# A shared square for own and left-hand attention scores, and who empties the turned banks

## The chip, the cores and the metric

One core of one Trainium2 chip runs the whole program in one launch. The metric is device time in microseconds from start to end of an execution, lower is better. Its engines work through queues of their own, in order, and wait for one another on semaphores only: TensorE (PE), VectorE (DVE), ScalarE (ACT), GpSimd (POOL) and SyncE (SP), which here issues the loads.

## The reference

Attention with a window and sinks, then two gated or mixing layers. Cut to what the change touches:

```python
scores = scale * np.matmul(q, k.transpose(0, 1, 3, 2))     # B=2, H=8, S=768, D=64
is_sink = pos[None, :] < int(n_sink)                       # n_sink = 4
rel = pos[:, None] - pos[None, :]
keep = is_sink | ((rel >= 0) & (rel < int(window)))        # window = 128
scores = np.where(keep, scores, -1000000000.0)
a = np.exp(scores - np.max(scores, axis=-1, keepdims=True))
a = a / (np.sum(a, axis=-1, keepdims=True) + 1e-09)
x = np.matmul(a, v)
# then h = relu(x @ w_in), halves u and v, v normalised, w_spatial @ v + b, u * v, @ w_out
# then a token mixer (w_tok1, w_tok2) and a channel mixer (w_ch1, w_ch2), each added to its input
```

Everything is float32. Products that need its precision are done as three products of a rounded high half and a low half (hi x hi, hi x lo, lo x hi); scores take the query once, with its halves stacked over the partitions, against k_hi and k_lo.

## The kernel before

**Tiles and heads.** The queries are cut into 12 tiles of 128 rows, six for each of the two sequences, and a tile has 8 heads: 96 heads in all, numbered n = 8t + h. In the text i is t modulo 6, the place in the sequence. A query of a tile can see its own tile's keys up to itself, keys of the tile to the left that lie after its own place (window 128), and the sinks. So a head scores 288 columns: 128 own, 128 left-hand, and 32 between them that hold the sinks. At i = 0 it scores only its own 128. The keys lie in `k_hi` and `k_lo` as two squares around the sink columns; even tiles overwrite the first, odd tiles the second, so own and left-hand change places from tile to tile.

**One head, step by step.** All engines walk the same numbered steps n, each with its own list for a step.
- TensorE, `score(n)`: two products (high and low keys) into one of two score banks; it waits until the mask step of head n-2 is done.
- VectorE, `mask_scores(n)` (L780): one fused step adds the mask to the bank, writes `masked` and takes the row's least value, since scores are negated. The profile shows it as a custom operation and an accumulator read.
- ScalarE, `exps(n)` (L611): exp(-(masked) + least) into `probs`.
- TensorE, `turn_pair(m)` at step 2m+3: transposes the squares of heads 2m and 2m+1 against the identity into one of two banks (L989). Two squares a head, so four transposes; at i = 0 one a head, so two.
- `pair_out(m)` copies the bank into `p_t`: ScalarE for even m (L627), VectorE for odd m (L788), 512 columns.
- TensorE, `values(m)` at step 2m+5: each square of `p_t` times 66 columns of V of its tile (64, a one for the sum, a zero), L1023. One such product shows as two records in the trace.
- Sinks: every fourth step ScalarE gathers the sink columns of four heads into `p_cat` (L619), TensorE turns them (L997) straight after the pair of odd m, ScalarE copies them out (L635), and one product adds their values (L1031).
- VectorE, `x_out(g)`, at steps divisible by 4, straight after the mask step: sum, reciprocal and product (L795, L797, L801) give `x_nat`.
- TensorE, `turn_x(t)` at step 8t+13: transposes x (L1005). ScalarE and VectorE split it into `x_hi` and `x_lo` (L642, L807).

**The two turn banks.** Pairs, sinks and x take them in turn, in the order of `TURNS`; before it writes a bank TensorE waits (`wait_turn_bank`) until what was turned two places earlier is copied out. In step 8t+13 the order is pair (odd m), sinks, x: x waits for the copy of that pair.

**Preparation.** For a group of four heads, ScalarE rounds the queries (`q_high`, L586) at n % 4 == 1 and VectorE makes their low halves (`q_low`, L769) at n % 4 == 2. The keys' high halves come from GpSimd (L515; the first two from ScalarE), their low halves from GpSimd (L517), both in `k_prepare` at n % 4 == 0, for the next group.

**Filler.** Quarters of the first layer's products (`first_quarters`, L950 to L952) are put between the attention's products on TensorE by the table `WINDOWS`, in units of four quarters: one unit in tiles 2 and 3, two in tiles 4, 5, 7, 8, 10 and 11, three in 6 and 9. ScalarE empties them (`first_out`). VectorE takes the moments of v at steps with n % 8 in (3, 7) and normalises it there, GpSimd takes the root and splits it (L548, L550). The order inside a step is written out by hand; there is no planner.

**After the attention** the rest of the filler, the spatial product, the output product and the two mixers run, TensorE-bound and with their own lines; the change does not touch them.

## Time and profile before

| | us |
|---|---|
| median of 3 runs (lowest to highest) | 509.32 (509.27 to 510.44) |
| the profiled execution | 509.37 |
| its span | 507.5 |
| TensorE busy | 492.1 (97%) |
| VectorE busy | 211.1 (42%) |
| ScalarE busy | 163.5 (32%) |
| GpSimd busy | 171.0 (34%) |

The span runs from the first to the last instruction; the execution's time has 1.9 us around it. The trace names engines PE (matmul), PEld (its weight load), DVE, ACT, POOL, SP. The number behind L is the line of the kernel. The granted TensorE clock is 0.999 on average. The shares are means over very different parts: in the attention part VectorE and ScalarE are two to four times as busy as behind it.

In a row of the timeline a span is an instruction's duration from start to end. Instructions of one engine overlap: the next can start before the end of the one in front, so what an instruction takes of its queue is the distance to the next start, where nothing is waited for.

### The profile page before, as it was taken

Reading aid. Unit: us, or ns where it says so; the run is one execution under the profiler, and the core shown is the slowest. Engines: PE = TensorE matmul, PEld = TensorE weight load, DVE = VectorE, ACT = ScalarE, POOL = GpSimd, SP = SyncE. Lnnn points to the kernel's source line nnn. Section 1 sums busy time; section 2 is a strip of 40 time slices with the busy share of each in tenths; the row PEclk is TensorE's granted clock in tenths of the full one; section 3 lists DMA queues with packets and bytes.
Section 4 is the critical chain, followed back from the end, with each engine's and each line's share of the span. In section 5 each row is a group of like instructions: output and inputs, shape, how many; then the busy total and the mean of one; then the engine's idle time right before and its main releaser. Section 6 shows DMA issues by size and latency. Waiting matters only on the chain.

```text
span 507.5 us, 7154 instructions
## 1 busy us (share of the span) xinstructions
PE 492.1 (97%) x2664; PEld 436.1 (86%) x2664; DVE 211.1 (42%) x527; ACT 163.5 (32%) x343; POOL 171.0 (34%) x185
## 2 busy tenths in 40 slices
PE   3899999999999999999999999999999999999997
PEld 2788989999999899999888898888888888888885
DVE  5577777677676416754222232112131131211212
ACT  5577656565556242112342232010010010010010
POOL 3655653654451488701305057970000000000000
PEclk9999999999999999999999999999999999999999
DMA  7455322432311134300202013420020000100002
GB/s 238 150 166 170 112 77 86 137 118 91 106 43 33 61 96 134 89 0 1 77 1 65 19 45 102 136 72 0 1 83 1 0 1 0 70 14 0 1 0 83
DMA packets 19189, 34.03 MB, mean 67 GB/s; under 512 B 2256, under 2 KB 4560, under 8 KB 19152
## 3 DMA queue, kind: packets, MB, share of 16 engines
q1 hardware_dynamic: 19008, 33.55, 21.1%
q8 instruction: 22, 0.36, 0.3%
q14 instruction: 15, 0.12, 0.1%
q10 hardware_dynamic: 144, 0.00, 0.0%
HBM read 30.39 MB, written 3.15 MB: 66 GB/s over the span
## 4 chain that ended last, share of the span: by engine, by line
PE 89%; POOL 4%; DMA 2%; DVE 2%; issue 2%; ACT 1%; SPq 0%; ACTq 0%; POOLq 0%; DVEq 0%
PE bank L950 24%; PE bank L951 24%; PE bank L952 24%; PE bank L1023 6%; PE bank L989 3%; PE bank L965 2%; PE bank L966 2%; PE bank L1031 1%; PE bank L1182 1%; PE bank L1005 1%; POOL win_lo L539 1%; POOL k_lo L517 1%; DMA stage<-w_in 1%; DMA stage<-w_sp 1%; POOL wsp_lo L539 1%
## 5 line engine op out<-in xcount | busy, mean ns | idle before, releaser
L939 DVE SCALAR_TENSOR_TENSOR hch_lo<-bank,hch_hi 128x512 fp32r<-128x512 f32 x36 | 24.9, 692 | 153.8 <-ACT hch_hi L728 153.8
L728 ACT ACTIVATE hch_hi<-bank 128x512 fp32r<-128x512 f32 x36 | 21.5, 598 | 169.0 <-PE bank L952 169.0
L611 ACT ACTIVATE probs<-masked,small 128x288 f32<-128x288 f32 (+1 forms) x96 | 49.0, 512 | 49.5 <-DVE small L780 49.2
L780 DVE CUSTOM_DVE_ANT_0 masked<-bank,masks 128x288 f32<-128x288 f32 (+1 forms) x96 | 41.0, 428 | 38.9 <-PE bank L966 33.8
L952 PE MATMUL bank<-up_hi,wc_lo 128*128 128x512 f32 x144 | 56.0, 389 | 0.0
L951 PE MATMUL bank<-up_lo,wc_hi 128*128 128x512 f32 x144 | 56.0, 389 | 0.0
L950 PE MATMUL bank<-hch_hi,wc_hi 128*128 128x512 f32 x144 | 56.0, 389 | 0.0
L951 PE MATMUL bank<-hch_lo,wc_hi 128*128 128x512 f32 x144 | 56.0, 389 | 0.0
L950 PE MATMUL bank<-up_hi,wc_hi 128*128 128x512 f32 x144 | 56.0, 389 | 0.0
L952 PE MATMUL bank<-hch_hi,wc_lo 128*128 128x512 f32 x144 | 56.0, 389 | 0.0
L1023 PE MATMUL bank<-v_sl,p_t 128*128 128x66 f32 x352 | 46.8, 276 | 0.0
L1023 PEld LDWEIGHTS bank<-v_sl,p_t 128*128 128x128 f32 x352 | 45.8, 199 | 0.4
L965 PE MATMUL bank<-k_hi,q_st 128*128 128x288 f32 (+1 forms) x96 | 35.4, 371 | 10.1 <-DVE q_st L769 8.0
L517 POOL TENSOR_TENSOR k_lo<-k_raw,k_hi 128x512 fp32r<-128x512 f32 x24 | 34.0, 1415 | 5.8 <-ACT k_hi L579 4.0
L950 PE MATMUL bank<-wsp_hi,vn_hi 128*128 128x384 f32 x96 | 32.1, 335 | 0.9 <-POOL vn_lo L550 0.9
L951 PE MATMUL bank<-wsp_lo,vn_hi 128*128 128x384 f32 x96 | 32.1, 334 | 0.0
L952 PE MATMUL bank<-wsp_hi,vn_lo 128*128 128x384 f32 x96 | 32.1, 334 | 0.0
L952 PEld LDWEIGHTS bank<-up_hi,wc_lo 128*128 128x128 f32 x144 | 27.0, 188 | 5.7
L952 PEld LDWEIGHTS bank<-hch_hi,wc_lo 128*128 128x128 f32 x144 | 27.0, 188 | 5.7
L950 PEld LDWEIGHTS bank<-hch_hi,wc_hi 128*128 128x128 f32 x144 | 27.1, 188 | 5.6
L951 PEld LDWEIGHTS bank<-up_lo,wc_hi 128*128 128x128 f32 x144 | 27.0, 188 | 5.6
L951 PEld LDWEIGHTS bank<-hch_lo,wc_hi 128*128 128x128 f32 x144 | 27.0, 188 | 5.6
(121 smaller groups left out, 1022.7 us busy)
## 6 DMA issues: line engine op xcount, KB each, us to landing
k_raw<-kT SPq DMA_DIRECT2D x24, 256.0 KB, 3.1
q_raw<-qT SPq DMA_DIRECT2D x24, 256.0 KB, 2.9
stage<-w_c SPq DMA_DIRECT2D x24, 256.0 KB, 2.7
v_sl<-vL SPq DMA_DIRECT2D x12, 264.0 KB, 2.9
outT<-out_sb SPq DMA_DIRECT2D x12, 256.0 KB, 2.1
stage<-w_sp SPq DMA_DIRECT2D x12, 192.0 KB, 2.5
stage<-w_in SPq DMA_DIRECT2D x8, 256.0 KB, 3.6
stage<-w_out SPq DMA_DIRECT2D x4, 256.0 KB, 3.2
```

Of the source, the lines that this page charges most:

```text
L517: pool.tensor_tensor(k_lo[:, hs, c0:c0 + P], raw, k_hi[:, hs, c0:c0 + P], ALU.subtract).then_inc(k_ready, 1)
L539: pool.tensor_tensor(lo, staged(n), hi, ALU.subtract).then_inc(w_lo_ready, 1)
L611: act.activation(probs[:, n % N_PROB, 0:w], masked[:, n % N_MASKED, 0:w], ACT.Exp, bias=least[:, n % 8:n % 8 + 1], scale=-1.0).then_inc(ex ...
L728: act.activation(hch_hi[:, u[2] % N_HCH, :], bank[:, :], ACT.Relu).then_inc(hi_ready, 1)
L780: dve.tensor_tensor_reduce(masked[:, n % N_MASKED, 0:w], score_bank[n % 2][:, 0:w], masks[:, m:m + w], 1.0, 3e38, ALU.add, ALU.min, least[ ...
L939: dve.scalar_tensor_tensor(out=hch_lo[:, f % N_HCH, :], in0=bank[:, :], scalar=0.0, in1=hch_hi[:, f % N_HCH, :], op0=ALU.max, op1=ALU.subt ...
L950: pe.matmul(out, a_hi, b_hi, start=first, stop=False, skip_group_check=skip)
L951: pe.matmul(out, a_hi, b_lo, start=False, stop=False, skip_group_check=skip)
L952: return pe.matmul(out, a_lo, b_hi, start=False, stop=last, skip_group_check=skip)
L965: pe.matmul(score_bank[n % 2][:, 0:w], q, k_hi[:, h, 0:w], start=True, stop=False)
L989: ins = pe.transpose(tr_bank[n % 2][:, at_:at_ + P], probs[:, head % N_PROB, c:c + P], ident[:, :])
L1023: ins = pe.matmul(bank[:, DV * place:DV * place + DV], p_t[:, m % N_PT, at_:at_ + P], v_sl[:, slot, DV * h:DV * h + DV], start=m % 2 == 0 ...
```

## The change

For the tiles with i of 2 and more, `merged(t)`, an entry of the square is own where the key lies at or below the query's place, and left-hand above: the two triangles fill one square exactly. The kernel after makes use of that.
- VectorE copies the own triangle over the left-hand square in the score bank (`copy_predicated`), waits for that on `own_placed`, and runs the fused mask step over the square and the sinks, 160 columns. ScalarE's exp has the same 160 columns.
- `turn_pair` turns one square per head. `pair_out(m)` is on ScalarE for every m and copies 256 columns. A step later VectorE writes, beside it in `p_t`, the square times a triangle of ones (`own_triangles`, SBUF to SBUF).
- `values(m)` multiplies the whole square by V of the left-hand tile and the own triangle by `v_diff`, own V minus left-hand V, which GpSimd makes (`value_difference`, twice a tile).
- At i = 1 the scores skip the sink columns: 256 in place of 288. There the turned bank holds four squares as before; VectorE copies the second head's (`second_head`), and ScalarE, after it, the first head's. At i = 0 ScalarE copies the 256 columns of every pair.
- The keys' high halves move from GpSimd to ScalarE, at n % 4 == 0, behind the other work of that step.
- Two triangles and a square mask are made at the start, and one mask fewer is written by ScalarE. Buffers are laid out anew.

```diff
@@ mask and slot geometry
+def merged(t):
+    return t % NT >= 2
+def in_bank(t):
+    i = t % NT
+    return slice(0, P) if i == 0 else slice(0, SLOT) if i == 1 else slice(0, P + SINKS) if i % 2 else slice(P, BAND)
+def squares(t):
+    i = t % NT
+    return [0] if i == 0 else [0, P] if i == 1 else [0] if i % 2 else [P]
+HALVED = [m for m in range(N_PAIR) if m // 4 % NT]
...
@@ gpsimd
-                if g >= 2:
-                    pool.wait_ge(s_k[g % 2], 16 * (g // 2 + 1))
-                    if g >= 4:
-                        pool.wait_ge(scored, 4 * (g - 1))
-                    pool.tensor_scalar(k_hi[:, hs, c0:c0 + P], raw, 1.0, 1.0, ALU.mult, ALU.mult).then_inc(k_high_done, 1)
...
+            def value_difference(t, half):
+                cols = slice(GV * half, GV * half + GV)
+                pool.wait_ge(s_v[t % 3], 16 * (t // 3 + 1))
+                pool.wait_ge(s_v[(t - 1) % 3], 16 * ((t - 1) // 3 + 1))
+                pool.wait_ge(valued, 4 * (t - 1) + 2 * half + 2)
+                pool.tensor_tensor(v_diff[:, cols], v_sl[:, t % 3, cols], v_sl[:, (t - 1) % 3, cols], ALU.subtract)\
+                    .then_inc(diff_ready, 1)
...
+                if n % 4 == 1 and (n // 8, n % 8 // 4) in diff_n:
+                    value_difference(n // 8, n % 8 // 4)
@@ scalar
             def pair_out(m):
-                cols = 2 * P * len(blocks(m // 4))
                 act.wait_ge(turned, turn_index[("pair", m)] + 1)
+                if m in halved_n and not merged(m // 4):
+                    act.wait_ge(pt_own, halved_n[m])
...
-                act.activation(p_t[:, m % N_PT, 0:cols], tr_bank[turn_index[("pair", m)] % 2][:, 0:cols], ACT.Copy)\
+                act.activation(p_t[:, m % N_PT, 0:2 * P], tr_bank[turn_index[("pair", m)] % 2][:, 0:2 * P], ACT.Copy)\
                    .then_inc(pt_act, 1)
...
-                for m in range(0, N_PAIR, 2):
+                for m in range(N_PAIR):
...
+                if n % 4 == 0 and 2 <= n // 4 + 1 < N_GROUP:
+                    k_high(n // 4 + 1)
@@ vector
+                if merged(t):
+                    own, previous = (odd, even) if t % 2 else (even, odd)
+                    dve.copy_predicated(previous, tri_own.bitcast(U32), own).then_inc(own_placed, 1)
                 if n >= N_MASKED:
                     dve.wait_ge(exped, n - N_MASKED + 1)
-                dve.tensor_tensor_reduce(masked[:, n % N_MASKED, 0:w], score_bank[n % 2][:, 0:w], masks[:, m:m + w],
+                if merged(t):
+                    dve.wait_ge(own_placed, placed_n[n])
+                dve.tensor_tensor_reduce(masked[:, n % N_MASKED, cols], bank[:, at_], masks[:, m:m + at_.stop - at_.start],
                                          1.0, 3e38, ALU.add, ALU.min, least[:, n % 8:n % 8 + 1]).then_inc(masked_ready, 1)
...
+            def second_head(m):
+                dve.wait_ge(turned, turn_index[("pair", m)] + 1)
...
+                dve.tensor_copy(p_t[:, m % N_PT, 2 * P:4 * P], tr_bank[turn_index[("pair", m)] % 2][:, 2 * P:4 * P])\
+                   .then_inc(pt_own, 1)
+            def own_triangles(m):
+                whole, own = p_t[:, m % N_PT, 0:2 * P], p_t[:, m % N_PT, 2 * P:4 * P]
+                dve.wait_ge(pt_act, m + 1)
+                dve.tensor_tensor(own.rearrange("p (h c) -> p h c", c=P), whole.rearrange("p (h c) -> p h c", c=P),
+                                  tri_turned.unsqueeze(1).to_broadcast([P, 2, P]), ALU.mult).then_inc(pt_own, 1)
...
-                for m in range(1, N_PAIR, 2):
-                    if turn_step(m) == n:
-                        pair_out(m)
+                for m in HALVED:
+                    if turn_step(m) == n and not merged(m // 4):
+                        second_head(m)
+                    if turn_step(m) == n - 1 and merged(m // 4):
+                        own_triangles(m)
@@ tensor
-                if kind == "pair" and m % 2 == 0:
-                    pe.wait_ge(pt_act, m // 2 + 1)
-                if kind == "pair" and m % 2 == 1:
-                    pe.wait_ge(pt_dve, m // 2 + 1)
+                if kind == "pair":
+                    pe.wait_ge(pt_act, m + 1)
...
+                pe.wait_ge(pt_act, m + 1)
+                if m in halved_n:
+                    pe.wait_ge(pt_own, halved_n[m])
+                if (t, g % 2) in diff_n and m % 2 == 0:
+                    pe.wait_ge(diff_ready, diff_n[t, g % 2])
...
+                    if t % NT == 0:
+                        parts = [(P * n, v_sl[:, t % 3, :])]
+                    elif t % NT == 1:
+                        parts = [(2 * P * n, v_sl[:, (t - 1) % 3, :]), (2 * P * n + P, v_sl[:, t % 3, :])]
+                    else:
+                        parts = [(P * n, v_sl[:, (t - 1) % 3, :]), (2 * P + P * n, v_diff)]
```

## Rows read from the trace of the kernel before

**Rows 1.** The page, chain of waits, shares of the span by engine.
```profile
PE 89%; POOL 4%; DMA 2%; DVE 2%; issue 2%; ACT 1%; SPq 0%; ACTq 0%; POOLq 0%; DVEq 0%
```

**Rows 2.** Busy time in one stretch: bounds, length, each engine's us (x instructions), clock, DMA.
```profile
50.60:64.10 13.50, 13.50 (x98) 12.56 (x97) 10.51 (x31) 9.00 (x20) 7.83 (x8) 1.00 0.36 117
```

**Rows 3.** Timeline, tile 10: start us, us, engine, line, operation, out<-in, shape, count.
```profile
141.00 0.30 PE L965 MATMUL bank<-k_hi,q_st 128*128 128x288 f32 x1
...
141.13 0.29 PE L966 MATMUL bank<-k_lo,q_st 128*128 128x288 f32 x1
...
141.96 0.60 PE L989 MATMUL bank<-ident,probs 128*128 128x128 f32 x4
...
142.39 1.00 PE L1023 MATMUL bank<-v_sl,p_t 128*128 128x66 f32 x8
```

**Rows 4.** Groups by form: xcount | busy us, mean ns | idle before, releaser.
```profile
L780 DVE CUSTOM_DVE_ANT_0 masked<-bank,masks 128x288 f32<-128x288 f32 x80 | 36.4, 455 | 32.2 <-PE bank L966 27.3 <-issue 4.3
...
L780 DVE CUSTOM_DVE_ANT_0 masked<-bank,masks 128x128 f32<-128x128 f32 x16 | 4.6, 290 | 6.7 <-PE bank L966 6.4
...
L611 ACT ACTIVATE probs<-masked,small 128x288 f32<-128x288 f32 x80 | 42.7, 534 | 41.9 <-DVE small L780 41.7
...
L611 ACT ACTIVATE probs<-masked,small 128x128 f32<-128x128 f32 x16 | 6.3, 398 | 7.5 <-DVE small L780 7.5
...
L627 ACT ACTIVATE p_t<-bank 128x256 f32<-128x256 f32 x4 | 1.5, 369 | 0.0
...
L515 POOL TENSOR_SCALAR k_hi<-k_raw 128x512 fp32r<-128x512 f32 x22 | 14.1, 639 | 36.1 <-PE bank L966 36.1
```

**Rows 5.** Timeline, tile 10, from scores of head 84 to the x transposes.
```profile
143.54 0.49 PE L965 MATMUL bank<-k_hi,q_st 128*128 128x288 f32 x1
...
144.20 0.46 DVE L780 CUSTOM_DVE_ANT_0 masked<-bank,masks 128x288 f32<-128x288 f32 x1 [1.56 <-PE bank L966]
...
144.58 0.16 DVE L795 TENSOR_SCALAR small<-bank 128x4 f32<-128x4 f32 x1
...
144.77 0.18 DVE L797 RECIPROCAL small<-small 128x4 f32<-128x4 f32 x1
...
144.98 0.42 DVE L801 TENSOR_TENSOR x_nat<-bank,small 128x256 f32<-128x256 f32 x1
...
145.33 0.45 DVE L780 CUSTOM_DVE_ANT_0 masked<-bank,masks 128x288 f32<-128x288 f32 x1
...
145.82 0.54 ACT L611 ACTIVATE probs<-masked,small 128x288 f32<-128x288 f32 x1 [0.38 <-DVE small L780]
...
145.94 0.69 DVE L788 COPY p_t<-bank 128x512 f32<-128x512 f32 x1 [0.16 <-PE bank L989]
...
146.26 0.26 ACT L635 ACTIVATE p_ts<-bank 128x128 f32<-128x128 f32 x1
...
146.69 0.65 PE L1005 MATMUL bank<-ident,x_nat 128*128 128x128 f32 x4
```

**Rows 6.** Timeline, tile 9, the same two instructions of TensorE.
```profile
128.66 0.49 PE L965 MATMUL bank<-k_hi,q_st 128*128 128x288 f32 x1
...
132.34 0.60 PE L1005 MATMUL bank<-ident,x_nat 128*128 128x128 f32 x4
```

**Rows 7.** Timeline, end of tile 8 and start of tile 9.
```profile
117.30 0.38 PE L965 MATMUL bank<-k_hi,q_st 128*128 128x288 f32 x1
...
121.39 0.46 DVE L780 CUSTOM_DVE_ANT_0 masked<-bank,masks 128x288 f32<-128x288 f32 x1
...
122.34 0.29 ACT L619 ACTIVATE p_cat<-probs 128x128 f32<-128x128 f32 x1
...
123.10 0.27 PE L997 MATMUL bank<-ident,p_cat 128*128 128x128 f32 x1
```

**Rows 8.** Timeline, start of tile 5, TensorE.
```profile
70.73 0.30 PE L997 MATMUL bank<-ident,p_cat 128*128 128x128 f32 x1 [0.42 <-ACT p_cat L619]
```

**Rows 9.** VectorE's low halves of the queries, min/median/max ns.
```profile
L769 DVE SCALAR_TENSOR_TENSOR q_st<-q_raw,q_st x24: 689/690/1079, 6.3 to 154.9; 64x512 fp32r<-64x512 f32 x24
```

More of the change, by code:

```diff
@@ L175 @@
 COLS = E_ID + P
-assert all(at % P == 0 for at in (A_V, A_PROBS, A_PT, A_PTS, A_CAT, A_X, B_X, X_SLOT, B_WIN, C_VN, D_U, E_V, E_STAGE, E_ID))
+assert H * DV <= 5 * P
+assert all(at % P == 0 for at in (A_V, A_DIFF, A_PROBS, A_PT, A_PTS, A_CAT, A_X, B_X, X_SLOT, B_WIN, C_VN, D_U, E_V, E_STAGE, E_ID))
 A_WSP = 0
@@ L210, in build @@
         banks = [ctx.enter_context(nc.psum_tensor(f"bank{i}", [P, 512], F32)) for i in range(8)]
-        k_hi = at("k_hi", A_K_HI, [H, BAND], F32R)
-        k_lo = at("k_lo", A_K_LO, [H, BAND], F32R)
+        k_hi_flat = at("k_hi", A_K_HI, [H * BAND + SINKS], F32R)
+        k_lo_flat = at("k_lo", A_K_LO, [H * BAND + SINKS], F32R)
+        k_hi, k_lo = (flat[:, 0:H * BAND].rearrange("p (h c) -> p h c", h=H) for flat in (k_hi_flat, k_lo_flat))
         q_st = at("q_st", A_Q, [2, 512], F32R)
@@ L219, in build @@
         vs_sl = at("vs_sl", A_VS, [2 * GV])
[L220 to L221 removed]
+        v_diff = at("v_diff", A_DIFF, [H * DV])
+        masked = at("masked", A_MASKED, [N_MASKED, SLOT])
+        probs = at("probs", A_PROBS, [N_PROB, SLOT])
         p_t = at("p_t", A_PT, [N_PT, 512])
@@ L227, in build @@
         scratch = at("mask_scratch", B_X + X_SLOT, [8, P])
-        rel_sb, key_sb, diag_keep, prev_keep, sink_keep, first_keep, second_keep = (scratch[:, i, :] for i in range(7))
+        rel_sb, key_sb, diag_keep, prev_keep, sink_keep, first_keep, second_keep, square_keep = (scratch[:, i, :] for i in range(8))
+        tri_own, tri_turned = masks[:, TRI_OWN:TRI_OWN + P], masks[:, TRI_TURNED:TRI_TURNED + P]
         x_hi = [at(f"x_hi{i}", B_X + X_SLOT * i, [KT, HALF], F32R) for i in range(2)]
@@ L959, in score @@
                     pe.wait_ge(k_ready, g + 1)
-                if h == 0 and t % NT == 1:
+                if h == 0 and t % NT == 2:
                     pe.wait_ge(ks_ready, t // NT + 1)
@@ L964, in score @@
                 q = q_st[:, g % 2, P * (n % 4):P * (n % 4) + P]
-                pe.matmul(score_bank[n % 2][:, 0:w], q, k_hi[:, h, 0:w], start=True, stop=False)
-                pe.matmul(score_bank[n % 2][:, 0:w], q, k_lo[:, h, 0:w], start=False, stop=True).then_inc(scored, 1)
+                high, low, out = k_hi[:, h, :], k_lo[:, h, :], score_bank[n % 2][:, 0:BAND]
+                if t % NT == 0:
+                    high, low, out = k_hi[:, h, 0:P], k_lo[:, h, 0:P], score_bank[n % 2][:, 0:P]
+                if t % NT == 1:
+                    high, low = beside_sinks(k_hi_flat, h), beside_sinks(k_lo_flat, h)
+                    out = score_bank[n % 2][:, 0:2 * P].rearrange("p (b c) -> p b c", b=2)
+                pe.matmul(out, q, high, start=True, stop=False)
+                pe.matmul(out, q, low, start=False, stop=True).then_inc(scored, 1)
             def wait_turn_bank(n):
@@ L987, in turn_pair @@
                     pe.wait_ge(exped, head + 1)
-                    for c, _ in blocks(m // 4):
+                    for c in squares(m // 4):
                         ins = pe.transpose(tr_bank[n % 2][:, at_:at_ + P], probs[:, head % N_PROB, c:c + P], ident[:, :])
@@ L1014, in values @@
                     pe.wait_ge(x_nat_ready, g - 1)
-                if m % 2 == 0:
-                    pe.wait_ge(pt_act, m // 2 + 1)
-                else:
-                    pe.wait_ge(pt_dve, m // 2 + 1)
-                at_ = 0
-                for head in (2 * m, 2 * m + 1):
-                    h, place = head % H, head % 4
-                    for _, slot in blocks(t):
+                pe.wait_ge(pt_act, m + 1)
[3 more added lines that the diff above has]
+                    pe.wait_ge(diff_ready, diff_n[t, g % 2])
+                first = m % 2 == 0
+                for n in range(2):
+                    h, place = (2 * m + n) % H, (2 * m + n) % 4
+                    if t % NT == 0:
+                        parts = [(P * n, v_sl[:, t % 3, :])]
[3 more added lines that the diff above has]
+                        parts = [(P * n, v_sl[:, (t - 1) % 3, :]), (2 * P + P * n, v_diff)]
+                    for at_, v in parts:
                         ins = pe.matmul(bank[:, DV * place:DV * place + DV], p_t[:, m % N_PT, at_:at_ + P],
-                                        v_sl[:, slot, DV * h:DV * h + DV], start=m % 2 == 0 and at_ == 0, stop=False,
-                                        skip_group_check=True)
-                        at_ += P
+                                        v[:, DV * h:DV * h + DV], start=first, stop=False, skip_group_check=True)
+                        first = False
                 if ("sink", g) in turn_index and m % 2:
```

78 lines of the change are left out of this document (43 added, 35 removed).

## Prediction

> **What bounds the kernel now.** I read the chain of waits first: TensorE holds 89% of it, VectorE 2% and ScalarE 1% [rows 1]. Whatever shortens TensorE's queue can therefore shorten the whole, as long as no other queue comes to release it. Next the table by stretches [rows 2]: the change touches the attention part alone, and there TensorE has no idle time (13.50 of 13.50 us around tile 4), while VectorE is busy for 10.51 and ScalarE for 9.00 us. So TensorE bounds, but VectorE's queue is full to 78%, and it works in a fixed order: it has little room to be late. The granted clock is 1.00 there, so I price nothing for the clock. The form table [rows 4] gives the durations, and three stretches of the timeline [rows 5 to 7] tell how close VectorE and ScalarE come to releasing TensorE. They are the part of the profile that decides here.
>
> **The change part by part.**
>
> *Transposes.* In the eight tiles with i from 2 to 5 (tiles 2 to 5 and 8 to 11) each head turns one square in place of two: 64 transposes go. Four of them take from 141.96 to 142.39 us on TensorE, 0.43 us, or 0.1075 each [rows 3]: 64 x 0.1075 = 6.9 us off. The value products stay at two a head, since the second now multiplies the own triangle by V_own minus V_prev. The tiles with i = 1 score 256 columns in place of 288, 32 products shorter by 32 columns each. A product of 288 columns releases the queue after some 0.13 us (141.00 to 141.13 us [rows 3]), so 32 columns are about 0.014 us and all 32 products 0.4 us. Half of them lie in the start phase, where TensorE waits anyway. I take 0.2. Together 7.1 us off, so 502.3 us is the floor if nothing new is waited for.
>
> *VectorE's mask step.* Before, one fused add and minimum over 288 columns, 0.455 us, after which the next instruction starts 0.38 us behind its start (144.20 to 144.58) [rows 4, 5]. Now a predicated copy of 128 columns within the score bank, a wait for it on the engine's own semaphore, then the fused step over 160 columns. The slope of the fused step is (455 - 290)/160 = 1.03 ns a column [rows 4], so 128 columns fewer take 0.13 us off: 0.38 becomes 0.25. No row shows a predicated copy, nor VectorE writing a bank. Bounds: 0.16 us, the time of an operation on four columns out of a bank, and 0.42, one of 256 columns out of a bank [rows 5]. The nearest row is the 128-column form of the fused step, also out of a bank, 0.29 [rows 4]. I take that, and 0.03 for the wait on itself (the gap in 144.58 + 0.16 to 144.77, where the next instruction waits in the same way). A mask step is then 0.32 + 0.25 = 0.57 in place of 0.38: 0.19 longer, 64 times.
>
> *Own triangles.* 32 products over 256 columns in SBUF take the place of 20 bank copies of 0.69 (two each in these eight tiles, 16 of the 20). The 256-column product at 144.98 takes 0.42 and lets the next start after 0.35 [rows 5]. VectorE as a whole: 8 x 0.19 + 4 x 0.35 - 2 x 0.60 = 1.7 us more a tile, 10.51 to 12.2 us against a tile of 13.50 - 0.86 = 12.6 for TensorE. It still fits in sum; what is lost is lost where the order makes TensorE wait.
>
> *ScalarE.* It gets 22 high halves of keys (from GpSimd, 0.64 each there [rows 4]), one more bank copy per four heads at 0.37 for 256 columns, and shorter exponentials (136 ns over 160 columns, so 0.11 less each [rows 4]). The key half is issued after exp(n) and the gather of a step n divisible by 4, 0.6 us before exp(n+1), which waits longer than that for VectorE's mask, so it is hidden. If VectorE were early it would cost up to 0.6 at each group. GpSimd gives up 14 us and gets 16 value differences; TensorE reads them a good four steps after they can start, so they are free.
>
> *The wait that I expect to bind: the x transposes.* In step 8t+13 TensorE turns pair, sinks and then x in alternate banks, so x waits until the pair's bank is emptied. Before, VectorE did that straight behind mask(n). Now ScalarE does it behind exp(n), which waits for mask(n). Walk through tile 10, n-1 = 84, n = 85 [rows 5]: mask(84) starts at 144.20 and takes 0.57, the own triangles 0.35, the three operations of x_out 0.75 as before (144.58 to 145.33), so mask(85) starts at 145.87 and not 145.33. Its fused step starts 0.32 later, at 146.19; exp(85) started 0.49 behind a fused step of 288 columns (145.33 to 145.82), so 0.36 behind this one: 146.55. ScalarE's next instruction came 0.44 behind exp (145.82 to 146.26), now 0.33: 146.88. + 0.37 bank copy = 147.25, + 0.06 (146.63 to 146.69) = 147.31. TensorE would otherwise be there at 146.69 - 0.22 = 146.47. Loss 0.84 us. All eight x turns of merged tiles have this order. Tile 9 has one more unit of filler: its x turn comes 132.34 - 128.66 = 3.68 us behind the start of the pair's scores, that of tile 10 after 146.69 - 143.54 = 3.15, so it loses 0.84 - 0.53 = 0.3 [rows 5, 6]. Sum 7 x 0.84 + 0.3 = 6.2 us.
>
> *Ends of tiles.* In the last two steps of a tile VectorE does two masks, x_lo, q_low and the moments. In tile 8 they keep it until mask(72) can start at 121.39 [rows 7]. It grows by 2 x 0.19 + 0.35 = 0.73, so mask(72) starts 121.39 - 117.30 + 0.73 = 4.82 us behind the scores of step 70. Gather ended 1.24 behind mask(72)'s start, now 0.19 - 0.11 more, 1.32: 6.14. TensorE wants the gathered columns 123.10 - 117.30 = 5.80 behind those scores, less 0.44 for four transposes: 5.36. Loss 0.8. Tile 10 has the same row pattern, 0.8. At the end of tile 4 it already waits 0.42 for the gather [rows 8]: there the delay of 0.81 is paid in full and the 0.44 aren't won, 1.25. Three ends with more cover (3, 5, 9) I put at 0.3 each. Sum 3.8 us.
>
> *Start.* Three of the key halves that leave GpSimd come before the filler starts, where GpSimd's low halves of weights set the pace; ScalarE gets the same work between its exponentials. Bounds -1.9 (three halves of 0.64 off GpSimd [rows 4]) and +1.9 (the same three on ScalarE); I take +0.3, since ScalarE's queue feeds the next scores.
>
> **Sum.** - 7.1 + 6.2 + 3.8 + 0.3 = + 3.2 us. The profiled execution took 509.37 us with a span of 507.5, and the median of the runs is 509.32, so one number serves both: 509.4 + 3.2 = **512.6 us**, slower by 0.6%.
>
> *A rule against the change.* Own triangles read two operands in SBUF. VectorE's q_low does that already: mostly 0.69 us, at worst 1.08 [rows 9]. The Trainium skill ("SBUF — State Buffer", section "SBUF: two separate sides") says that such an operation and a GpSimd one that reads SBUF take a shared port pair in turn, and that the loser blocks for the whole instruction; what it gives is a rival, below.
>
> **Rivals.**
>
> A, no change (508.8 to 510.4). Only the x turns cost, the tile ends have cover that I don't see in [rows 7]: 509.4 - 7.1 + 6.2 + 0.3 = 508.8, with one end paid 509.6. For it: VectorE has time left over in sum. Against: [rows 7, 8] show it late at the ends already.
>
> B, faster, about 506.7. The predicated copy is at its lower bound of 0.16: 0.13 less per mask, 2 x 8 masks before x turns and 3 x 6 at tile ends, 34 x 0.13 = 4.4, which gives 508.2, and the start wins 1.2 net of the key halves. It decides from a copy under some 0.2 us. For it: GpSimd is relieved where the start needs it. Against: the 128-column row at 0.29 [rows 4].
>
> C, slower by more, 516 to 517. The own triangles lose their slot to GpSimd or the copy takes 0.42: 34 x 0.13 = 4.4 gives 517.0. If GpSimd holds it back as it does q_low, a product of own triangles waits up to 0.39 (1.08 - 0.69 [rows 9]) in the 14 places where it is on the path; with GpSimd at work in two thirds of them 9 x 0.39 = 3.5, 516.1. For it: the long rows of q_low. Against: at the x turn GpSimd now waits for ScalarE's key half, so it is mostly idle there. The port rule of that page is this case, at the price that the rows allow.
>
> D, the transposes go but the order never binds (x finds its bank free): 502.3 to 504. It would need mask(85) to end 0.84 us sooner than the walk, which no row supports.
>
> **How the numbers follow.** Forecast 0.42, A 0.19, B 0.15, C 0.18, D 0.06. The range from 505.0 to 517.5 leaves out D and the far side of C, and takes both ends of the unknown copy; the forecast's own is 511 to 514.5. A measurement of this kernel tells 0.3%, 1.5 us, from no change: faster (under 507.8) 0.22, same 0.20, slower (over 510.9) 0.58.
>
> **What would show it.** In the profile after: 112 transposes of probs and not 176, at 0.11 us each; a predicated copy near 0.29, 64 times; TensorE waiting for ScalarE's copy of p_t ahead of the x transposes, some 0.8 us, seven or eight times; waits for p_cat at starts of tiles 5, 9 and 11; key halves on ScalarE beside no wait of TensorE for k_lo. I am wrong if x transposes follow the value products without a gap, if the copy is far from 0.3, or if the stretch before 29 us moves by over 1.2 us.

## The result, and the profile after

| | before | after |
|---|---|---|
| median (lowest to highest), us | 509.88 (509.27 to 510.88) | 524.15 (523.89 to 524.64) |
| span of the profiled execution | 507.5 | 522.3 |
| TensorE busy | 492.1 | 496.0 (95%) |
| VectorE busy | 211.1 | 221.6 (42%) |
| mean granted clock | 0.999 | 0.993 |

The ratio is 1.028 [1.026, 1.030]: slower by 14.3 us, or 14.8 by span, where 3.2 were forecast. The sign held; the size did not, and the time lies outside the range.

The chain of waits after, shares by engine; VectorE had 2% in [rows 1].

```profile
PE 80%; DVE 11%; issue 4%; ACT 2%; DMA 2%; POOL 0%; DVEq 0%; SPq 0%; ACTq 0%
```

So VectorE's queue now holds some 57 us of that chain (11% of 522) in place of 10. The stretches of the profile after say where TensorE lost time: bounds, length, busy us of PE, PEld, DVE, ACT and POOL, granted clock, DMA share, GB/s. In [rows 2] PE was never idle at clock 1.00.

```profile
43.00:56.00 13.00, 10.86 (x64) 8.86 (x63) 8.07 (x34) 7.62 (x21) 6.83 (x7) 0.95 0.30 93
56.00:70.00 14.00, 12.85 (x79) 11.22 (x77) 11.68 (x40) 8.19 (x21) 6.57 (x6) 0.92 0.29 87
70.00:84.00 14.00, 13.57 (x82) 12.46 (x82) 10.40 (x34) 6.89 (x19) 7.26 (x8) 0.88 0.18 60
```

TensorE is idle for 2.1 of 13 us around tile 3. The clock figures are means of two levels: in the trace it goes to the lower one, 1.2 GHz, twice, for 3.4 us each, at 54.7 and at 71.8 us. The length of each tile, from the start of its first scores to the next tile's (the last: to head 95), read off the two timelines:

| tile | 0 | 1 | 2 | 3 | 4 | 5 | 6 | 7 | 8 | 9 | 10 | 11 |
|---|---|---|---|---|---|---|---|---|---|---|---|---|
| before | 9.7 | 12.1 | 12.2 | 12.5 | 13.9 | 14.6 | 13.6 | 11.6 | 13.2 | 15.9 | 13.9 | 11.5 |
| after | 9.4 | 13.4 | 13.1 | 16.3 | 16.8 | 15.0 | 14.1 | 11.4 | 14.7 | 16.5 | 15.1 | 13.1 |

The eight merged tiles carry 12.9 us of the 14.1, tiles 3 and 4 alone 6.6. From head 95 to the first spatial product it is 0.7 us more (25.1 before, 25.8 after), and from that product on nothing changed (320.5 and 320.6). What TensorE waits for in the attention (engine, line, releaser; us in all, times, longest). The PEld rows are the weight load's side of the same waits, so they don't add to the PE rows; "issue" means that the profile shows no releaser:

```profile
PEld bank L1074 <- issue: 9.0, 13, 1.4
PE bank L1074 <- ACT p_cat L667: 5.9, 9, 1.1
PEld bank L1082 <- ACT p_t L677: 4.5, 8, 0.9
PE bank L1082 <- ACT p_t L677: 3.4, 7, 0.8
```

L1074 is the transpose of the gathered sinks, L1082 that of x. The x transposes wait seven times, as forecast, six times for 0.40 to 0.48 us and once for 0.78; the gather costs more than they do, where before its waits made 0.7 us in two places, one of them in [rows 8]. The added work by form:

```profile
L834 DVE COPY_PREDICATED bank<-masks,bank 128x128 f32<-128x128 uint32 x64 | 18.6, 291 | 21.7 <-PE bank L1045 21.1
L839 DVE CUSTOM_DVE_ANT_0 masked<-bank,masks 128x160 f32<-128x160 f32 x64 | 20.8, 325 | 10.0 <-DVE bank L834 1.1
L854 DVE TENSOR_TENSOR p_t<-p_t,masks 128x256 f32<-128x256 f32 x32 | 15.4, 480 | 0.5 <-ACT p_t L677 0.4
L821 DVE SCALAR_TENSOR_TENSOR q_st<-q_raw,q_st 64x512 fp32r<-64x512 f32 x24 | 20.5, 855 | 3.1 <-ACT q_st L635 2.4
L628 ACT ACTIVATE k_hi<-k_raw 128x512 fp32r<-128x512 f32 x24 | 14.8, 616 | 1.9 <-DMA k_raw<-kT 1.9
```

The copy takes 0.29 us as priced. But VectorE stands idle for 10.0 us ahead of the 64 fused steps. The timeline of tile 10's step with the x transpose, after, against [rows 5]:

```profile
155.28 0.49 PE L1044 MATMUL bank<-k_hi,q_st 128*128 128x288 f32 x1
...
155.93 0.29 DVE L834 COPY_PREDICATED bank<-masks,bank 128x128 f32<-128x128 uint32 x1
...
156.37 0.33 DVE L839 CUSTOM_DVE_ANT_0 masked<-bank,masks 128x160 f32<-128x160 f32 x1
...
157.70 0.29 DVE L834 COPY_PREDICATED bank<-masks,bank 128x128 f32<-128x128 uint32 x1
...
158.13 0.32 DVE L839 CUSTOM_DVE_ANT_0 masked<-bank,masks 128x160 f32<-128x160 f32 x1
...
158.50 0.43 ACT L659 ACTIVATE probs<-masked,small 128x160 f32<-128x160 f32 x1 [0.61 <-DVE small L839]
...
158.83 0.36 ACT L677 ACTIVATE p_t<-bank 128x256 f32<-128x256 f32 x1
...
159.25 0.66 PE L1082 MATMUL bank<-ident,x_nat 128*128 128x128 f32 x4 [0.43 <-ACT p_t L677]
```

Every link of the walk is there, in order. The x transpose starts 3.97 us behind the scores, where 3.77 were walked. The difference is in the step from copy to fused step: 0.44 and not 0.32, twice. In 62 of the 64 heads it is 0.42 to 0.44; the other two, 0.78 and 0.86, stay unexplained. The next runs are about that, and about what the rest costs.

### The profile page after: what moved, and what is told of

It is laid out like the page before. It is cut to its first block, busy times and chain, and to the rows that moved or that the text cites. A ratio compares the mean times of both kernels' runs of the same rounds, so it can differ in the third digit from the quotient of the medians.

```text
span 522.3 us, 7207 instructions
## 1 busy us (share of the span) xinstructions
PE 496.0 (95%) x2600; PEld 433.2 (83%) x2600; DVE 221.6 (42%) x608; ACT 169.5 (32%) x386; POOL 168.8 (32%) x179
## 4 chain that ended last, share of the span: by engine, by line
PE 80%; DVE 11%; issue 4%; ACT 2%; DMA 2%; POOL 0%; DVEq 0%; SPq 0%; ACTq 0%
PE bank L1019 22%; PE bank L1021 22%; PE bank L1020 22%; PE bank L1107 5%; DVE masked L839 2%; DVE q_st L821 2%; DVE bank L834 2%; PE bank L1044 2%; PE bank L1082 1%; PE bank L1045 1%; PE bank L1066 1%; PE bank L1265 1%; DVE p_t L854 1%; DMA stage<-w_sp 1%; DVE small L881 1%
## 5 line engine op out<-in xcount | busy, mean ns | idle before, releaser
L659 ACT ACTIVATE probs<-masked,small 128x160 f32<-128x160 f32 (+2 forms) x96 | 41.9, 436 | 61.0 <-DVE small L839 59.6
L553 POOL TENSOR_TENSOR k_lo<-k_raw,k_hi 128x512 fp32r<-128x512 f32 x24 | 30.6, 1274 | 73.5 <-ACT k_hi L628 69.4
L1044 PE MATMUL bank<-k_hi,q_st 128*128 128x288 f32 (+2 forms) x96 | 35.9, 375 | 10.7 <-DVE q_st L821 8.7
L839 DVE CUSTOM_DVE_ANT_0 masked<-bank,masks 128x160 f32<-128x160 f32 (+2 forms) x96 | 32.0, 335 | 24.6 <-PE bank L1045 11.6
L1107 PE MATMUL bank<-v_sl,p_t 128*128 128x66 f32 x224 | 39.7, 286 | 0.5 <-DVE p_t L854 0.3
L1107 PEld LDWEIGHTS bank<-v_sl,p_t 128*128 128x128 f32 x224 | 34.9, 208 | 3.1 <-issue 1.1
L1044 PEld LDWEIGHTS bank<-k_hi,q_st 128*128 128x128 f32 x96 | 20.1, 209 | 14.9 <-issue 7.1
```

The costliest lines, as they stand in the source:

```text
L553: pool.tensor_tensor(k_lo[:, hs, c0:c0 + P], raw, k_hi[:, hs, c0:c0 + P], ALU.subtract).then_inc(k_ready, 1)
L659: act.activation(probs[:, n % N_PROB, cols], masked[:, n % N_MASKED, cols], ACT.Exp, bias=least[:, n % 8:n % 8 + 1], scale=-1.0).then_inc( ...
L839: dve.tensor_tensor_reduce(masked[:, n % N_MASKED, cols], bank[:, at_], masks[:, m:m + at_.stop - at_.start], 1.0, 3e38, ALU.add, ALU.min, ...
L1044: pe.matmul(out, q, high, start=True, stop=False)
L1107: ins = pe.matmul(bank[:, DV * place:DV * place + DV], p_t[:, m % N_PT, at_:at_ + P], v[:, DV * h:DV * h + DV], start=first, stop=False, s ...
```

## The experiments

All ratios are against the kernel before, run on the same chip. A gain or loss in us is the difference of two medians. The kernel before itself had medians from 509.29 to 510.37 on these chips, so a difference between runs of different chips can be off by some 0.5 to 1 us. Against the kernel before on its own chip, the change lost 14.3 us, run 3 10.0, run 4 5.6, run 8 7.1 and run 11 6.2.

**1. The saving alone** (before, merged tiles turn one square a head).

```diff
-                    for c, _ in blocks(m // 4):
+                    for c, _ in blocks(m // 4)[0:1 if m // 4 % NT >= 2 else 2]:
```

> The kernel before, with one change: in the tiles with i of 2 and more each head turns one square instead of two (64 transposes fewer). The banks are still copied in their full 512 columns and all four value products are made, so the second square's product works on old data: that part of the computation is left out. Theory (TensorE bounds, and what it saves comes back): 64 x 0.1075 = 6.9 us off, 509.9 to 503.0 us. Rival (the transposes were hidden behind the other engines anyway): 508 us or more. If VectorE and ScalarE hold TensorE at some places even so, it lies between, near 505.

506.49 us, ratio 0.994 [0.993, 0.996]: 3.2 us, under half of 6.9, and between the expectation's two theories. TensorE, done sooner, now waits for the gather four times, 2.0 us, where it was 0.7 in two:

```profile
PE bank L997 <- ACT p_cat L619: 2.0, 4, 0.9
```

The old kernel was bound by TensorE, but its feeders were hardly earlier.

**2. Without the copy and its wait** (the left-hand scores stay in place of the own).

```diff
-                    dve.copy_predicated(previous, tri_own.bitcast(U32), own).then_inc(own_placed, 1)
...
-                if merged(t):
-                    dve.wait_ge(own_placed, placed_n[n])
```

> The kernel after without the predicated copy and the wait for it: the mask step is the fused operation over 160 columns alone, the own scores are left out of the square. The trace of after shows 0.44 us from the start of that copy to the start of the fused step (0.32 predicted), 64 times. Theory (the lengthened mask step is what makes VectorE late, and TensorE waits for what follows it): most of the 14 us go, 524.2 to 508 or less (505 if TensorE is back to back again). Rival (the key halves and bank copies on ScalarE hold it): at most 4 us off, 520 or more. Rival (the own triangles' products and GpSimd's port): 515 to 518.

509.75, ratio 1.000 [0.999, 1.001]: 14.4 us better than the change, which is the whole loss. But the copy isn't the only cost: against run 1, which also turns fewer squares, 3.3 us remain. GpSimd is in part of them: TensorE waits for the own triangles four times, 1.3 us in all. One of them:

```profile
147.93 1.29 POOL L594 TENSOR_TENSOR vn_lo<-v_sb,vn_hi 128x512 fp32r<-128x512 f32 x1
148.03 0.08 DVE L836 DVE_READ_ACCUMULATOR2_ANT small<- 128x1 f32 x1
148.03 1.47 DVE L851 TENSOR_TENSOR p_t<-p_t,masks 128x256 f32<-128x256 f32 x1
...
149.65 0.41 PE L1104 MATMUL bank<-v_sl,p_t 128*128 128x66 f32 x2 [0.36 <-DVE p_t L851]
```

The own triangles take 1.47 us in place of 0.42: they start behind GpSimd's product of two SBUF operands and end 0.28 us after it (149.22), and TensorE waits for them. The Trainium skill ("SBUF — State Buffer", section "SBUF: two separate sides") describes this lock, taken for a whole instruction; the row agrees.

**3. ScalarE's bank copy ahead of its exponential** in merged tiles.

```diff
+                for m in range(N_PAIR):
+                    if turn_step(m) == n and merged(m // 4):
+                        pair_out(m)
...
-                    if turn_step(m) == n:
+                    if turn_step(m) == n and not merged(m // 4):
```

> The kernel after, with ScalarE's copy of the turned bank ahead of exp(n) in the step, not behind it, in the tiles with i of 2 and more. Theory (x transposes wait for the copy, which waits for exp and so for the mask): the 7.9 us of waits at the x transposes nearly go, since the copy can be done 0.7 us earlier; 524.2 to 518 or so, if the exponentials, 0.37 us later where ScalarE is behind, do not make the gather later. Rival (VectorE's queue decides wherever one looks, the x wait only takes over from the next wait): 523 to 525.

519.72, ratio 1.020 [1.018, 1.021]: 4.4 us back. The waits of the x transposes for `p_t` are gone and the clock is 1.000; the gather's are 6.7 us, where the change had 5.9, and the value products now wait for ScalarE's copy three times, 1.6 us. So the x term was real, at about 4.4 where 6.2 were forecast.

**4. The copy beside the scores, without a wait** (its result isn't used).

```diff
-                    dve.copy_predicated(previous, tri_own.bitcast(U32), own).then_inc(own_placed, 1)
+                    dve.copy_predicated(bank[:, BAND:BAND + P], tri_own.bitcast(U32), own).then_inc(own_placed, 1)
...
-                if merged(t):
-                    dve.wait_ge(own_placed, placed_n[n])
```

> The kernel after, with the predicated copy written to unused columns of the same bank, and the fused step not waiting for it: the copy's own time stays, the engine's wait for its result goes (the own scores are left out of the square). After shows 0.44 us from start to start, 0.29 of it the copy. Theory (the wait is 0.12 us longer than I priced and on the path in over 30 places): 524.2 to 517 to 519; the copy then takes 0.2 or so of the queue. Rival (the copy's own time is the whole price): 522 or more, and with the 509.8 of the run without a copy that splits the 14 us between copy and wait.

514.93, ratio 1.012 [1.010, 1.013]. Of the 14.4 us of run 2 the wait is 9.2 and the copy 5.2; with the kernel before of each chip taken off they are 8.6 and 5.6. The fused step now starts 0.20 us behind the copy's start in 49 heads, and 0.33 in the 15 whose copy follows the low halves of the queries directly.

**5. The copy into SBUF, wait kept.** The destination is `u_sb[:, 1, 3, S - P:S]`.

> The kernel after with the predicated copy written to unused columns of SBUF and not into the bank, the wait for it kept (the own scores are left out of the square). The wait cost 0.15 us behind the end of the copy and not the 0.03 I priced; the 0.03 came from writes to SBUF. Theory (it is writing the bank that makes the wait long): start to start falls from 0.44 to 0.32, and the time by 64 x 0.12 = 7.7 us of queue at 0.6, to 519 or 520. Rival (a wait for a 128-column copy costs that much wherever it writes): 0.44 and 524.

524.37, ratio 1.029 [1.027, 1.030]; still 0.44 from start to start. That it writes a score bank is not the cause.

**6. A plain copy, wait kept.**

```diff
-                    dve.copy_predicated(previous, tri_own.bitcast(U32), own).then_inc(own_placed, 1)
+                    dve.tensor_copy(previous, own).then_inc(own_placed, 1)
```

> The changed kernel with a plain copy in place of the predicated one (all 128 columns of every row are placed, so the scores are not the reference's); the wait for it stays. Theory 1, the late release belongs to the predicated copy (its wait lasts some 0.15 us behind the copy's end, where waits behind other instructions of this queue lasted 0.03): the fused step then starts 0.32 us behind the copy's start and not 0.44, 64 x 0.12 = 7.7 us of VectorE's queue, of which 0.6 counted in the run without the wait: -4.6 us, about 519.5. Theory 2, any operation that writes the score bank or is as short as this one releases its own engine as late: still 0.44, and 523.5 to 524.5.

525.82, ratio 1.030 [1.027, 1.033], 0.44 again. Nor is it the predicated form.

**7. A one-column copy takes the wait.**

```diff
                     dve.wait_ge(own_placed, placed_n[n])
+                    dve.tensor_copy(u_sb[:, 1, 3, S - 1:S], bank[:, 0:1])
```

> The changed kernel with a copy of one column (out of the score bank into SBUF) between the wait and the fused step, which so has a plain instruction ahead of it and no wait of its own for the copy. Theory 1, the fused step as the waiter is what pays (a wait ahead of it lasts 0.15 us behind the releasing instruction's end, and 0.03 ahead of ordinary ones): the small copy starts 0.32 us behind the predicated copy's start, the fused step some 0.06 to 0.1 behind that, 0.38 to 0.42 in all, and the time is 522 to 524. Theory 2, any instruction that waits for a 128-column operation on the bank starts as late: the small copy starts at 0.44, the fused step at 0.50 to 0.54, 64 x 0.08 x 0.6 = 3 us slower, about 527.

523.27, ratio 1.027 [1.024, 1.029]. The small copy starts 0.38 to 0.40 behind the predicated one in all 64, nearer to 0.44 than to 0.32, and the fused step 0.08 later. The waiting instruction isn't it either, or only by some 0.05.

**8. The wait for exp ahead of the copy**, so that one wait is left between the two.

```diff
                 if merged(t):
+                    if n >= N_MASKED:
+                        dve.wait_ge(exped, n - N_MASKED + 1)
...
-                if n >= N_MASKED:
+                if n >= N_MASKED and not merged(t):
```

> The changed kernel with the wait for the exponential (which frees the slot of masked) moved ahead of the predicated copy in merged tiles, so that one wait is left between copy and fused step. Theory 1, the second wait at this place is what takes the 0.12 us: 0.32 start to start, and about 519.5. Theory 2, it has long been served and costs nothing: still 0.44, and 523.5 to 524.5.

517.47, ratio 1.014 [1.012, 1.017]: 6.7 us back by moving a wait that had always been served. The timeline of this run:

```profile
147.67 0.30 DVE L836 COPY_PREDICATED bank<-masks,bank 128x128 f32<-128x128 uint32 x1 [0.82 <-PE bank L1047]
148.00 0.32 DVE L841 CUSTOM_DVE_ANT_0 masked<-bank,masks 128x160 f32<-128x160 f32 x1
```

0.33, and 0.31 to 0.34 in all 64: the 0.32 of the prediction. The profile after shows what was different (a line of the kernel, DVEq for VectorE's sequencer; count; min/median/max ns):

```profile
L838 DVEq EVENT_SEMAPHORE  x64: 21/21/21, 30.9 to 177.6; - x64
```

L838 is the wait for the copy. It became an instruction of its own, 64 times, while the wait for exp, written ahead of it, stands alone 28 times, all outside the merged tiles. The Trainium skill ("Perfetto Trace Analysis", section "Identifying Dependency Chains") says that an instruction that waits on multiple engines may get such instructions in front; the trace agrees with its 64, where one of the two engines is the instruction's own. In run 8 the exp wait has them and the wait for the copy none:

```profile
L834 DVEq EVENT_SEMAPHORE  x64: 21/21/1215, 28.9 to 170.8; - x64
```

The starts of these rows show where the 0.12 lies. In the kernel after, the separate wait starts 0.32 to 0.34 us behind the copy's start in all 64 heads, where in run 8 the fused step itself starts, and the fused step follows it 0.11 later (in 62 of them). Runs 5, 6 and 7 left this separate wait where it was (64 in each), so none of them could show this; in run 7 it stands ahead of the small copy, which starts 0.06 behind it.

Two waits as such are not dear: `x_nat` has two from tile 2 on, and starts 0.03 behind the reciprocal's end in all 24 instances, before and after. There it is the other, served wait that stands alone, and it starts 0.01 behind the reciprocal's start, so it is over before the reciprocal is:

```profile
L867 DVEq EVENT_SEMAPHORE  x20: 21/21/21, 45.0 to 185.1; - x20
```

So the 0.12 goes with a separate wait for the engine's own last result. That writing the two waits in the other order would do the same as run 8 follows from this, but wasn't tried.

**9. Copy and wait on the kernel before**, all else kept; the same without the wait.

```diff
+                if t % NT >= 2:
+                    dve.copy_predicated(score_bank[n % 2][:, BAND:BAND + P], ident[:, :].bitcast(U32),
+                                        score_bank[n % 2][:, 0:P]).then_inc(own_placed, 1)
...
+                if t % NT >= 2:
+                    dve.wait_ge(own_placed, sum(e // H % NT >= 2 for e in range(n + 1)))
```

> The kernel before, all its transposes and bank copies kept, with the predicated copy of 128 columns (into unused columns of the score bank, so the result is the reference's) and the wait for it ahead of the fused step in the 64 heads of merged tiles. Each mask step gets 0.44 us longer (0.29 copy + 0.15 wait). Theory 1, VectorE's queue sets the steps wherever an x transpose or a tile's end needs it (the 34 places of the prediction): 34 x 0.44 = 15 us, 524 to 526, the same as the whole change, although no transpose went. Theory 2, the kernel before has cover in each tile (VectorE 10.5 of 13.5 us), and 8 x 0.44 = 3.5 us a tile just eats it: under 517.

> The same without the wait: each mask step gets 0.20 us longer. Theory 1: 34 x 0.20 = 6.8 us, 516 to 517. Theory 2, cover: 510 to 512. Against the run with the wait it also gives the price of the wait at the old kernel's place: 0.24 x 64 = 15.4 us of queue, of which the changed kernel paid 9.2.

518.92, ratio 1.018 [1.016, 1.021], and 512.43, 1.004 [1.003, 1.006], against 510.16: 8.8 and 2.3 us. Both lie nearer to theory 2, cover, but above its figures: of the 28 us put into VectorE's queue 31% comes out at the end, of 12.8 a fifth. The first 0.2 us of a mask step nearly fit into the old kernel's cover, the next 0.24 cost 6.5. So the price of one more microsecond in that queue is not one factor: it rises as the cover is used up.

**10. Runs 3 and 4 together.**

> The changed kernel with two edits that were run alone before: ScalarE's bank copies ahead of its exponential (-4.4 us), and the predicated copy put beside the scores without the wait (-9.2 us; the copy's result is not used, so the scores of the later square are left out). Theory 1, the two lateness terms are paid in different places (x transposes here, tile ends there): they add, 524.15 - 13.6 = 510.5. Theory 2, both shorten one chain (mask, exponential, copy or gather, transpose), and what one has removed the other can't remove again: 512.5 to 514.5. Theory 3, the gaps of TensorE go, and with them its half-speed stretches and restarts: under 509.5.

515.51, ratio 1.011 [1.009, 1.013], run 4 within its uncertainty. They don't add: what run 3 won was lateness that the mask step had caused. That is theory 2, though its 512.5 to 514.5 was still too low.

**11. No product for the own triangles** (the second product takes the whole square).

> The kernel after without the own triangles' product: the second value product takes the whole square as well, so that part of the computation is left out. Theory: 32 x 0.35 us of VectorE's queue and all waits for the port in it go, so 516 to 518. If only the port waits mattered (2 us of the 15.4 us busy), 522.

515.53, ratio 1.013 [1.010, 1.015]: 8.6 us, about as much as the wait (run 4, on the same chip, has 514.93).

**12. The triangles elsewhere.** Between copy and fused step, on GpSimd, or (with run 3) a step later:

> The kernel after, with VectorE's own triangles issued between the predicated copy and the fused step of the mask, where the engine otherwise waits 0.15 us for its own copy; before they came behind the fused step. Theory (VectorE's queue is what is too long): 32 x 0.15 us less in the queue, of which what lies on the path comes back: 520 to 522. Rival (the mask of an even step itself is what is late, its result now comes 0.25 us later): 525 or more.

> The kernel after, with the own triangles' products made by GpSimd, ahead of its other work of a step. VectorE's queue loses 32 x 0.35 us and its exposure to GpSimd's port in that product. Theory (VectorE's queue decides): 0.35 us off at each of the 8 x turns and each of the tile ends, 524.2 to 518 or less, if GpSimd (24 us more for it) is in time. Rival (the shared port: one more GpSimd operation in each pair of steps blocks VectorE's q_low): 522 to 528, with long q_low rows.

> The kernel after with two reorderings: ScalarE's bank copy ahead of exp(n), as in the second experiment on order, which gave 519.7; and VectorE's own triangles behind the mask of the odd step, one step later, so that they no longer stand between mask(n) of an even step and mask(n+1). Theory (what counts is how late mask(n+1) of the first pair of a group is): 0.35 us off at x turns and gathers, some 16 places, 519.7 to 514 to 516, if TensorE's value products do not wait for the triangles in their place. Rival (VectorE's total is what counts): 519 to 520.

524.02 (ratio 1.030 [1.028, 1.031]), 532.35 (1.044 [1.040, 1.048]) and 569.51 (1.119 [1.117, 1.121]). The first fills the wait in some 25 heads (the next instruction starts 0.19 to 0.23 behind the copy) but wins nothing: the triangles take 585 ns on average there (480 in the change), VectorE waits 1.7 us for ScalarE's copies, which was 0.4, and TensorE waits for the gather 14 times, 9.3 us, in place of 9 times and 5.9. The fused step comes later in those heads, as the rival said. On GpSimd the triangles come too late for TensorE, and they hold VectorE's q_low up (mean 1008 ns, 855 in the change):

```profile
PE bank L1108 <- POOL p_t L559: 12.6, 10, 2.8
...
142.44 0.74 POOL L559 TENSOR_TENSOR p_t<-p_t,masks 128x256 f32<-128x256 f32 x1
...
142.66 1.06 DVE L831 SCALAR_TENSOR_TENSOR q_st<-q_raw,q_st 64x512 fp32r<-64x512 f32 x1
```

The 12.6 us of direct waits are the larger part; the expectation had made them a condition ("if GpSimd is in time") and priced only q_low. A step later on VectorE, the value products wait for them, far longer than I had expected:

```profile
PE bank L1110 <- DVE p_t L857: 30.6, 20, 2.4
```

**13. Key halves and value difference.** The high halves back on GpSimd (from the kernel after), or on ScalarE in the kernel before; and no `v_diff` (own V used).

> The kernel after, with the keys' high halves back on GpSimd as before (22 instructions of 0.64 us there, 0.62 on ScalarE). Theory (VectorE's mask step decides): within 1.5 us of 524.2, perhaps a gain of 1 at the start. Rival (ScalarE's longer queue is the cause): 515 to 519.

> The kernel before with one part of the change alone: the keys' high halves on ScalarE. Putting them back on GpSimd in the kernel after cost 7.3 us, and its trace has longer q_low rows on VectorE (0.96 us mean against 0.86). Theory (each GpSimd operation that reads SBUF lengthens VectorE's two-operand ones): q_low falls from 0.79 to 0.70 to 0.75 us mean, and the kernel wins 0.5 to 1.5 us. Rival (the seven microseconds came from the start or from GpSimd's lateness in the longer kernel): no change, or slower by the 0.6 us that ScalarE then takes in each group.

> The kernel after without GpSimd's value differences (16 operations, 13.6 us there); the second product takes the own values instead, so that part of the computation is left out. Theory of the shared port: VectorE's q_low and triangle rows get shorter (0.86 and 0.48 us mean now, 0.69 and 0.42 without GpSimd), 2 to 3 us of VectorE's queue, of which 0.5 to 0.6 per us lie on the path: 522.5 to 523. Rival (GpSimd's work moves no one): 524.

531.5 (1.042 [1.041, 1.044]), 509.34 (0.999 [0.999, 1.000]) and 523.73 (1.027 [1.025, 1.030]). Moving the key halves is worth 7.3 us in the new kernel and nothing in the old one; in the new one both the theory (within 1.5 us) and the rival (faster) missed. With them on GpSimd VectorE's products of two SBUF operands take longer (q_low mean 962 ns against 855, triangles 573 against 480) and TensorE's waits for them and for ScalarE's copies grow (10.3 against 8.7 us, 5.4 against 3.4). That the shared port alone does this is argued from these rows, not separated from GpSimd's later work. My expectation that q_low would get faster in the old kernel missed: mean 830 ns, 787 before. The value differences are free within the uncertainty, as priced, though the triangles get shorter without them (462 ns).

## Why the prediction missed

**The step that failed** is in *VectorE's mask step*: "and 0.03 for the wait on itself", from the gap behind an ordinary self-wait. The copy (0.29) and the fused step (0.25) were right. The wait lasts 0.12 longer, since the fused step had a wait already and the new one became an instruction of its own, which starts when the copy's result is there and puts the fused step 0.11 behind itself. The mask step is 0.69, not 0.57: 0.31 over before and not 0.19. Run 8 takes only that away and wins 6.7 us. The profile of before could have warned: there the wait for exp already stands as such an instruction 92 times, and I read no sequencer rows:

```profile
L779 DVEq EVENT_SEMAPHORE  x92: 21/21/1928, 11.0 to 161.9; - x92
```

**The transposes** are gone as forecast (112 at 0.11), but run 1 shows that they bring 3.2 us and not 6.9. An engine that finishes sooner meets its feeders sooner: the eight merged tiles got shorter by 0.2 to 0.8 us each, where 0.86 was due, and 0.7 of the 4.4 us won by head 95 were lost again before the first spatial product. I had counted that at the x turns and the ends alone.

The two can't be added up to the 11.6 us by which the span missed. Part of the 3.7 us stood in the sum under other names: 0.22 at each of eight x turns and 0.44 at three tile ends for TensorE's earlier arrival, 3.1 us. And they were measured in different kernels, where, as run 10 shows, such terms need not add. What is shown is that the mask step's longer wait is worth 6.7 us, over half of the miss.

**The x transposes** were late in the way that was walked, seven times, but their waits are 3.4 us in all, some 0.43 each where 0.84 was priced. Run 3 puts the term at 4.4 in place of 6.2.

**The ends of tiles.** Of the gather's nine waits, 5.9 us, five lie at ends of tiles and make 2.7 us, where 3.8 was forecast. The two that were walked came out: 0.76 and 0.78 for 0.8. The end of tile 4, put at 1.25, has no wait at all, nor has that of tile 3. The other four, 3.2 us, lie in x steps, 0.99, 1.15 and 0.75 of them in tiles 3 to 5, ahead of the x transpose in the same step, for which I had no gather term at all. The 0.12 of each mask step explain part of it.

**Rival C's mechanism** came true beside the forecast: GpSimd's two-operand work stretches the triangles (mean 480 ns, worst 949, against 416) and q_low (worst 1.73 us, against 1.08 [rows 9]). Of the triangles' 15.4 us busy, though, the stretch is only 2.0 (32 times 64 ns); most of them is their own place in the queue. Run 11 gives 8.6 us for the triangles as a whole. I had priced them by VectorE's mean load ("it still fits in sum"), and gave this case 0.18.

**The clock** I priced at nothing. In the kernel after TensorE's clock falls to its lower level twice, from 54.7 to 58.1 us and from 71.8 to 75.2 us. Ahead of the first TensorE waited 0.99 us (to 52.8) and 0.43 (to 54.6), ahead of the second 1.15 (to 69.2) and 0.43 (to 71.0). Behind the 0.75 and 0.40 us of tile 5 (to 85.6 and 87.3) it doesn't fall. The timeline after shows products of 512 columns at both levels:

```profile
57.22 0.63 PE L1021 MATMUL bank<-win_hi,x_lo 128*128 128x512 f32 x1
...
59.93 0.40 PE L1020 MATMUL bank<-win_lo,x_hi 128*128 128x512 f32 x1
```

Two stretches of 3.4 us at half the rate are 3.4 us of full clock, but only a part of it seems to lie on the path. Of the four executions of the kernel after, the one with mean clock 0.997 took 523.89 us, the two with 0.993 took 524.15 and 524.16, the one with 0.990 took 524.64: 0.75 us for 0.007 of clock, which is 3.7 us of full clock. In run 8 the two executions at 0.996 took 1.2 us more than the two at 0.999. From these two slopes I estimate 0.7 to 2.6 us of the loss; no run changed the clock alone.

**The start** is 0.9 us longer (head 16 at 29.9 in place of 29.0) for 0.3; in the other runs of the changed order it scatters from 28.4 to 31.0, and in the two of run 9 it is 28.4 and 30.4, so I don't explain it.

**What stays open:** the split of the rest between clock, port and start. No version here beats the kernel before except run 1, which leaves squares out. Run 8 is the best form of the change: 517.47, still 1.4% slower. Run 8 together with run 3's order wasn't tried. Its two remaining costs on VectorE are the 64 copies (5.2 us between runs 2 and 4) and the 32 triangle products, whose removal from the change won 8.6 us in run 11.

## What to carry to other kernels

When an edit adds a wait, look at which waits the instruction has already and which of them becomes an instruction of its own in the sequencer's rows; put the wait for the engine's own last result on the instruction itself, and the served one ahead of other work. In the four places looked at here (the mask step before and after, the copy of run 8, `x_nat`) the wait written later in the kernel was the one that stood alone. Before moving work off the bounding engine onto a queue that feeds it, add a dummy of that size to the old kernel: here 0.20 us a step cost 2.3 us, and 0.44 cost 8.8. A saving on the bounding engine is worth its price only as far as its feeders have room.

## What the hardware showed that I had not expected

- A predicated copy of 128 columns takes 0.29 us within a bank and 0.30 into SBUF. Without a wait the next instruction starts 0.20 behind its start in 49 of 64 cases (0.33 in 15); with one own wait on it 0.32; with that wait as an instruction of its own 0.44. A separate wait that is served already costs nothing that shows (0.03 in 24 of 24).
- GpSimd's two-operand products hold up VectorE's: 1.47 us for 0.42 beside a GpSimd product of 1.29.
- Twice, behind waits of TensorE of 0.99 and 0.43 and of 1.15 and 0.43 us, the granted clock went to 1.2 GHz for 3.4 us; a 512-column product then took nearly twice as long to give way (0.43 against 0.23 us).
